# Splitting the first chunk's x right behind attention, and multiplying its rms norm in behind the gate product and h

## The reference

```python
attn = softmax(mask(q @ k.T / 8)); x = attn @ v          # heads 0-3: last 32 keys; 4-7: every 32nd key
rms = sqrt(mean(x * x, -1) + 1e-6)
xn = x / rms * rms_g
g = xn @ w_gate                                          # 512 x 1536
x = (g / (1 + exp(-g)) * (xn @ w_val)) @ w_out           # 1536 x 512
logits = x @ gate + modality_bias[modality_id]           # 8 experts, top 1
out = prob * (relu(x @ w1[e]) @ w2[e])
```

## Time and profile before

| | us |
|---|---|
| median of 3 runs | 973.58 (973.51 to 975.59) |
| the profiled execution | 974.21 |
| its span in the trace | 972.5 |
| TensorE busy | 895.7 |
| DVE, ACT, POOL busy | 434.2, 375.2, 314.7 |

### The profile page before, as it was taken

The page is one execution under the profiler, slowest core; times in us unless marked ns, Lnnn a source line. Parts: engine busy times, 40 slices in busy tenths (PEclk is TensorE's granted clock), DMA queues, the critical chain, the costliest instruction groups (busy, mean ns, idle before and its releaser), DMA issues.

```text
span 972.5 us, 15470 instructions
## 1 busy us (share of the span) xinstructions
PE 895.7 (92%) x5270; PEld 772.6 (79%) x5270; DVE 434.2 (45%) x1120; ACT 375.2 (39%) x952; POOL 314.7 (32%) x375
## 2 busy tenths in 40 slices
PE   6869999999999998999999999992599999999996
PEld 5647888888878886889899989982488888888885
DVE  4644544533454334432533252227374665453651
ACT  4654653544554345521221321122253443333430
POOL 2543575224423442254234222221211222222220
PEclk9999999999999998999999999995699999999999
DMA  9931321321214200211121111112653556242420
GB/s 217 260 98 39 96 50 49 91 70 57 60 33 121 58 23 22 66 33 44 33 76 33 44 65 44 33 34 109 238 209 113 185 205 212 78 161 90 151 98 24
DMA packets 68644, 90.46 MB, mean 93 GB/s; under 512 B 38557, under 2 KB 42653, under 8 KB 68576
## 3 DMA queue, kind: packets, MB, share of 16 engines
q1 hardware_dynamic: 64896, 78.31, 26.5%
q0 software_dynamic: 3680, 11.28, 3.5%
HBM read 80.13 MB, written 10.22 MB: 93 GB/s over the span
## 4 chain that ended last, share of the span: by engine, by line
PE 84%; DVE 6%; ACT 4%; issue 2%; DMA 2%; POOL 1%; SPq 0%; DVEq 0%; POOLq 0%; ACTq 0%
PE ps L718 32%; PE ps L755 13%; PE ps L1272 12%; PE ps L1293 12%; PE ps L670 3%; PE ps L699 3%; PE ps L646 2%; PE ps L1304 2%; PE ps L680 2%; PE ps L775 1%; PE ps L1281 1%; DMA w_raw<-in_moe_w 1%; ACT sm L859 1%; PE ps L766 1%; ACT L865 1%
## 5 line engine op out<-in xcount | busy, mean ns | idle before, releaser
L1001 DVE SCALAR_TENSOR_TENSOR h<-h,ps 128x384 f32<-128x384 f32 x72 | 39.9, 554 | 191.5 <-ACT h L882 191.5
L553 POOL TENSOR_TENSOR sm<-sm,rinv 72x288 f32<-72x288 f32 (+1 forms) x52 | 51.7, 994 | 223.2 <-DVE rinv L964 223.1
L718 PE MATMUL ps<-x_hi,gate_hi 128*128 128x384 f32 x288 | 105.8, 367 | 4.7 <-DVE h L1001 4.7
L718 PE MATMUL ps<-x_hi,val_hi 128*128 128x384 f32 x288 | 102.7, 356 | 0.0
L718 PE MATMUL ps<-x_hi,gate_lo 128*128 128x384 f32 x288 | 98.7, 343 | 0.0
L718 PE MATMUL ps<-x_lo,gate_hi 128*128 128x384 f32 x288 | 98.6, 342 | 0.0
L718 PE MATMUL ps<-x_lo,val_hi 128*128 128x384 f32 x288 | 97.2, 338 | 0.0
L718 PE MATMUL ps<-x_hi,val_lo 128*128 128x384 f32 x288 | 97.1, 337 | 0.0
L581 POOL CAST out_hi<-out_raw 128x512 fp32r<-128x512 f32 x72 | 45.8, 636 | 154.8 <-DMA out_raw<-in_moe_w_out 154.8
L583 POOL TENSOR_TENSOR out_lo<-out_raw,out_hi 128x512 fp32r<-128x512 f32 x72 | 93.6, 1300 | 5.8
L755 PE MATMUL ps<-out_hi,h_hi 128*128 128x512 f32 x216 | 89.7, 415 | 2.4 <-DVE h_lo L1012 2.4
(11 more groups left out here) (196 smaller groups left out, 1908.1 us busy)
## 6 DMA issues: line engine op xcount, KB each, us to landing
w_raw<-in_moe_w SPq DMA_DIRECT2D x64, 512.0 KB, 7.2
out_raw<-in_moe_w_out SPq DMA_DIRECT2D x72, 256.0 KB, 2.6
x_rows<-y_tiles SPq DMA_DIRECT2D x18, 256.0 KB, 2.4
gate_raw<-in_moe_w_gate SPq DMA_DIRECT2D x4, 768.0 KB, 7.0
val_raw<-in_moe_w_val SPq DMA_DIRECT2D x4, 768.0 KB, 7.0
qk<-in_q SPq DMA_DIRECT2D x8, 288.0 KB
qk<-in_k SPq DMA_DIRECT2D x8, 288.0 KB
vstr<-in_v SPq DMA_DIRECT2D x8, 288.0 KB
```

The costliest lines, as they stand in the source:

```text
L553: pool.tensor_tensor(s3, s3, rinv[0:n, i, :].unsqueeze(2).to_broadcast([n, 4, c]), ALU.mult).then_inc(s_no, 1)
L718: mm = pe.matmul(ps[:, bank, 0:CH], w[:, i, kk, cols], x[:, kk, :], start=(kk == 0 and n == 0), stop=(kk == KT - 1 and n == 2))
L1001: dve.scalar_tensor_tensor(out=hf[n % 2][:, :], in0=hf[n % 2][:, :], scalar=1.0, in1=ps[:, 0, 0:CH], op0=ALU.add, op1=ALU.mult).then_inc(s ...
```

## The change

For the first chunk alone, x isn't normalised. Right behind the evacuation of O (ticks 8, 12, 14, 15) ACT casts xT times the gain to x_hi and DVE subtracts to x_lo. The norm goes into a tile of its own (nr_0) and DVE multiplies it in twice per step of chunk 0: on the gate product ahead of tanh (norm_gate), and on h (in form_h). The early stretch has 16 ticks, so the turn of group 13, values 12 and 13 and all behind lie beside products; O of groups 12 to 15 goes to bank 7, the scores of groups 12 to 15 all use banks 5 and 6, and the sum of squares is made at the start of val's product of f = 0, with the norm chain one tick later. The pairs of x are taken in the order 2, 3, 0, 1 everywhere. The gain's load has a semaphore of its own.

```diff
-EARLY = 18
+EARLY = 16
-SS = {0: EARLY - 2, **{c + 1: at(c, 9, 2) for c in range(NC - 1)}}
+SS = {0: at(0, 0, 1), **{c + 1: at(c, 9, 2) for c in range(NC - 1)}}
+X_SPLIT_0 = {2: 8, 3: 12, 0: 14, 1: 15}
+X_SPLIT_AT = by_tick((kk, s) for kk, s in X_SPLIT_0.items())
...
         def score_banks(j):
-            return 0 if SCORE[j] < EARLY and j % 2 else 5
+            return 0 if j < HEAD - 4 and j % 2 else 5
...
             def score(j):
-                elif j >= 2:
-                    pe.wait_ge(s_m, 4 * j - 4)
+                else:
+                    former_user = max((i for i in range(j) if score_banks(i) == bank), default=-1)
+                    if former_user >= 0:
+                        pe.wait_ge(s_m, 4 * former_user + 4)
...
             def product(bank, wh, wl, f, half, done, new=None):
-                for kk in range(half * KT // 2, (half + 1) * KT // 2):
+                for o in range(half * KT // 2, (half + 1) * KT // 2):
+                    kk = ORDER[o]
...
             def gate_product(c, f, half):
                     if c == 0 and f == 0:
-                        pe.wait_ge(s_m, 4 * SCORED[EARLY])
+                        pe.wait_ge(s_m, 4 * (HEAD - 4))
...
+            def x_split_0(kk):
+                if kk == ORDER[0]:
+                    act.wait_ge(s_gain, 16)
+                act.wait_ge(s_oe, last_of_first_chunk(kk) + 1)
+                act.activation(xh[:, kk, :], xT[:, kk, x_cols(0)], ACT.Copy,
+                               scale=rms_gain[:, kk:kk + 1]).then_inc(s_xh, 1)
...
             def tanh(n):
+                if n < FT:
+                    act.wait_ge(s_si, n + 1)
+                    if n:
+                        act.wait_ge(s_gf, n)
+                    act.activation(th_0[:, :], hf[n % 2][:, :], ACT.Tanh, scale=0.5).then_inc(s_th, 1)
+                    return
...
-                if (sub, half) == (1, 0):
+                if (sub, half) == ((2, 0) if (c, f) == (0, 0) else (1, 0)):
                     tanh(FT * c + f)
...
                 for j in EXPS_AT.get(s, []):
                     exps(j)
-                if s == EARLY - 1:
-                    x_split(0)
+                for kk in X_SPLIT_AT.get(s, []):
+                    x_split_0(kk)
...
+            def x_split_0(kk):
+                dve.wait_ge(s_xh, ORDER.index(kk) + 1)
+                dve.scalar_tensor_tensor(out=xl[:, kk, :], in0=xT[:, kk, x_cols(0)], scalar=rms_gain[:, kk:kk + 1],
+                                         in1=xh[:, kk, :].bitcast(f32), op0=ALU.mult,
+                                         op1=ALU.subtract).then_inc(s_xl, 1)
...
+            def norm_gate(n):
+                dve.wait_ge(s_g, n + 1)
+                if n >= 2:
+                    dve.wait_ge(s_hl, n - 1)
+                    dve.wait_ge(s_y, n - 1)
+                dve.tensor_tensor(hf[n % 2][:, :], ps[:, 0, 0:CH], nr_0[:, :], ALU.mult).then_inc(s_si, 1)
+            def form_gate(n):
+                dve.wait_ge(s_th, n + 1)
+                dve.scalar_tensor_tensor(out=hf[n % 2][:, :], in0=th_0[:, :], scalar=1.0, in1=hf[n % 2][:, :],
+                                         op0=ALU.add, op1=ALU.mult).then_inc(s_gf, 1)
...
             def form_h(n):
-                dve.wait_ge(s_si, n + 1)
+                dve.wait_ge(s_gf if n < FT else s_si, n + 1)
...
+                if n < FT:
+                    formed.then_inc(s_hn, 1)
+                    dve.wait_ge(s_hn, n + 1)
+                    formed = dve.tensor_tensor(hf[n % 2][:, :], hf[n % 2][:, :], nr_0[:, :], ALU.mult)
+                formed.then_inc(s_hf, 1)
...
                 if (sub, half) == (1, 0):
-                    scale_gate(FT * c + f)
+                    if c:
+                        scale_gate(FT * c + f)
+                    elif f:
+                        norm_gate(f)
+                if (c, sub, half) == (0, 1, 1):
+                    if f == 0:
+                        normalise_x(0)
+                        norm_gate(0)
+                    else:
+                        form_gate(f)
                 if (sub, half) == (2, 0):
+                    if (c, f) == (0, 0):
+                        form_gate(0)
                     form_h(FT * c + f)
...
                 for val, i in SPLIT_AT.get(s - 1, []):
                     w_lo(val, i, splits)
-                if s == EARLY - 1:
-                    x_split(0)
+                for kk in X_SPLIT_AT.get(s, []):
+                    x_split_0(kk)
```

More of the change, by code:

```diff
@@ L404, in last_batch, with last_of_first_chunk @@
             return (CH * c + CH - 1) // S
+        def last_of_first_chunk(kk):
+            return max(i for i, (hp, g) in enumerate(GROUPS) if hp == kk and (hp >= 2 or g < 2))
         def step_of(s):
@@ L556, in square @@
             def square(c, kk):
[L558 to L561, removed]
+                last = NG * last_batch(c) + LAST[kk] if c else last_of_first_chunk(kk)
+                pool.wait_ge(s_oe, last + 1)
+                if c == 1 and kk == ORDER[0]:
+                    pool.wait_ge(s_n3, 1)
+                elif c and kk == ORDER[0]:
+                    pool.wait_ge(s_xn, KT * (c - 1))
                 x = xT[:, kk, x_cols(c)]
@@ L713, in product @@
                 i, cols = f // QF, slice(f % QF * P, (f % QF + 1) * P)
-                for kk in range(half * KT // 2, (half + 1) * KT // 2):
+                for o in range(half * KT // 2, (half + 1) * KT // 2):
+                    kk = ORDER[o]
                     if new is not None:
-                        pe.wait_ge(s_xl, KT * new + kk + 1)
+                        pe.wait_ge(s_xl, KT * new + o + 1)
                     for n, (w, x) in enumerate(((wh, xh), (wh, xl), (wl, xh))):
                         mm = pe.matmul(ps[:, bank, 0:CH], w[:, i, kk, cols], x[:, kk, :],
-                                       start=(kk == 0 and n == 0), stop=(kk == KT - 1 and n == 2))
+                                       start=(o == 0 and n == 0), stop=(o == KT - 1 and n == 2))
                 if half:
@@ L868, in root @@
                 act.activation(nr[:, :], nr[:, :], ACT.Exp, scale=-0.5).then_inc(s_root, 1)
+            def x_split_0(kk):
[4 more added lines that the diff above has]
+                               scale=rms_gain[:, kk:kk + 1]).then_inc(s_xh, 1)
             def x_split(c):
[L871 to L874, removed]
+                act.wait_ge(s_vp, FT * c)
+                for o, kk in enumerate(ORDER):
+                    act.wait_ge(s_xn, KT * (c - 1) + o + 1)
                     act.activation(xh[:, kk, :], xT[:, kk, x_cols(c)], ACT.Copy).then_inc(s_xh, 1)
             def tanh(n):
+                if n < FT:
[4 more added lines that the diff above has]
+                    return
                 act.wait_ge(s_g, n + 1)
@@ L983, in normalise_x @@
                 dve.wait_ge(s_n2, c + 1)
-                dve.scalar_tensor_tensor(out=nr[:, :], in0=nt[:, :], scalar=1.5, in1=nr[:, :],
+                dve.scalar_tensor_tensor(out=(nr if c else nr_0)[:, :], in0=nt[:, :], scalar=1.5, in1=nr[:, :],
                                          op0=ALU.add, op1=ALU.mult).then_inc(s_n3, 1)
                 dve.wait_ge(s_n3, c + 1)
-                for kk in range(KT):
+                for kk in ORDER if c else ():
                     x = xT[:, kk, x_cols(c)]
@@ L990, in normalise_x @@
                                              in1=nr[:, :], op0=ALU.mult, op1=ALU.mult).then_inc(s_xn, 1)
+            def x_split_0(kk):
[3 more added lines that the diff above has]
+                                         op1=ALU.subtract).then_inc(s_xl, 1)
             def x_split(c):
[L993 to L994 removed]
+                for o, kk in enumerate(ORDER):
+                    dve.wait_ge(s_xh, KT * c + o + 1)
                     dve.tensor_tensor(xl[:, kk, :], xT[:, kk, x_cols(c)], xh[:, kk, :].bitcast(f32),
                                       ALU.subtract).then_inc(s_xl, 1)
+            def norm_gate(n):
[8 more added lines that the diff above has]
+                                         op0=ALU.add, op1=ALU.mult).then_inc(s_gf, 1)
             def scale_gate(n):
@@ L1004, in form_h @@
             def form_h(n):
-                dve.wait_ge(s_si, n + 1)
+                dve.wait_ge(s_gf if n < FT else s_si, n + 1)
                 dve.wait_ge(s_vp, n + 1)
-                dve.scalar_tensor_tensor(out=hf[n % 2][:, :], in0=hf[n % 2][:, :], scalar=0.5, in1=ps[:, 1, 0:CH],
-                                         op0=ALU.mult, op1=ALU.mult).then_inc(s_hf, 1)
+                formed = dve.scalar_tensor_tensor(out=hf[n % 2][:, :], in0=hf[n % 2][:, :], scalar=0.5,
+                                                  in1=ps[:, 1, 0:CH], op0=ALU.mult, op1=ALU.mult)
+                if n < FT:
[3 more added lines that the diff above has]
+                formed.then_inc(s_hf, 1)
             def h_split(n):
```

19 lines of the change are left out of this document (12 added, 7 removed).

## The result

The changed kernel takes 984.75 us (median of 4 runs, 983.39 to 985.68), the kernel before 973.81 in the same comparison: ratio 1.0107, interval 1.0093 to 1.0120. That is +10.9 us where +5.2 was forecast, outside the range.

A forecast was written before the change was run, and what follows sets the result against it. TensorE, busy 92% of a 972.5 us span, was taken as the bound. 2.9 up to f = 1, 2.0 for the clock and 0.3 for chunk 0's rest gave +5.2 us, 978.8 us, range 974.3 to 981.8.

The forecast's parts named there:

- Part 1: Early stretch, ticks 8 to 15: new splits delay DVE's copies at ticks 9 and 13, +2.2 us each, 4.4 in all.
- Part 2: Early stretch two ticks shorter: sum of squares starts at 75.35, where it was 61.88, and no longer waits for POOL.
- Part 3: Norm beside f = 0's products: DVE's chain releases the q/k turn ahead of f = 1 at 87.7 against 84.82, +2.9 us.
- The wait for norm_t: TensorE ahead of values 15: val half 0 covers 2.0 of 3.2 us, 1.2 stay idle.
- Part 4: TensorE clock: f = 1 starts at 1.2 GHz after bursts with gaps; slow products cost +2.0 us.
- The number of slow products: In f = 1: 14 products at the slow clock, 0.15 us more each.
- The upper bound: Clock cost at most 3.4 us, for 23 slow products, as from 72.3 to 80.3 in the kernel before.
- the first rival: Clock rises inside f = 0, near 73.5: +1.8 us in all, 975.4; chance 0.17.
- Part 5: Chunk 0 behind f = 1: two DVE multiplications per step, h 0.6 us later, +0.3 us over eleven steps.
- The early rise of the clock: Clock up inside f = 0: clock term 0, +2.9 becomes +1.5, total 975.4; chance 0.17.
- The absorbed waits: Early waits at ticks 9 and 13 never reach TensorE: 4.4 us back, +0.8, 974.4; chance 0.18, not slower.
- DVE as the bound of chunk 0: Norm on h, two SBUF inputs beside POOL, delays each maximum: +6 over +5.2, 984.5; chance 0.10.

The follow-up runs named there:

- experiment 1: Kernel after with DVE's four early subtractions (x_lo) at the end of the next tick, behind copies and maximum: 978.49 us, ratio 1.0035.
- experiment 7: Kernel after with gate_lo for f = 3 behind the maximum of group 17, not ahead of form_gate of f = 0: 984.40 us, ratio 1.0108.
- experiment 2: Kernel after with 12 and 14 unused products put into TensorE's two waits, ahead of values 15 and the turn before f = 1: 983.15 us, ratio 1.0081.
- experiment 3: Kernel after with chunk 1's four multiplications of x behind the norm on the gate product of f = 10: 982.79 us, ratio 1.0077.
- experiment 4: Kernel after without the norm on chunk 0's gate from f = 1 on, norm on h kept, output different: 977.94 us, ratio 1.0025.
- the four kernels: Kernel after with three, five, four or seven instruction moves on DVE, ACT and TensorE: 974.34, 973.88, 974.84, 973.93 us; ratios 0.9977, 0.9979, 0.9994, 0.9992.
- the kernel of five moves: Kernel after with x_lo, weight splits, chunk 1's multiplications and values 15 later, and the step-end maximum ahead of h_lo: 973.88 us, ratio 0.9979.
- that of three moves: Kernel after with early x_lo a tick later, weight splits two ticks later, chunk 1's multiplications behind f = 10's gate norm: 974.34 us, ratio 0.9977.

## Why the prediction was right in direction and wrong in size

*Part 1, the early waits (+4.4).* Right, in place and size: the copies came at 35.82 and 51.52 (forecast 36 and 51.3), and experiment 1 gives 5.3 us back, 4.8 for the two and the rest for ticks 14 and 15. The second wait is the longer one, since that subtraction took 0.96 us and not 0.6.

*Part 2.* Right. The first product at 66.13 (65.5), the sum of squares at 75.55 (75.4), without POOL.

*Part 3 (+2.9).* Measured 2.6, and DVE was the late one. Inside it one term was wrong: gate_lo was taken at 1.75 us on the path, experiment 7 shows 0.5, since ACT's tanh comes from behind the exponentials and would have been late by itself. That the sum came out so near was in part luck: a path that it didn't have ends only 0.5 us ahead of the one it had. The wait for norm_t was 2.44 and not 1.2, because the clock had risen: val's first product started 0.46 us behind the start of the sum of squares, and val half 0 was through 1.52 us later, at 77.53.

*Part 4, the clock (+2.0).* Mechanism right, 2.8 us measured, 2.7 of it by experiment 2; with experiment 3's execution it would be 1.4, so the size is not a fixed one. The number of slow products, 14, was met: from 87.86 to 93.17. The upper bound counted 23 such products ahead of 80.3 in the kernel before, where its rows have 18, so it should have been 2.7 and not 3.4. The course was another one: I had it low throughout, it rose in f = 0 (the first rival's condition) and fell again behind the waits. That rival's result, a faster f = 1, did not come. The Trainium skill (TensorE: Matmul & The Clock Gate, "HAM oscillation — how this bites in real kernels") describes this: waits between bursts make the clock fall and each new burst pays for it. The rows agree in part: with the waits filled the level stays (experiment 2), but not every wait of 2.4 us or more made it fall (last section).

*Part 5, the rest of chunk 0 (+0.3).* This is the step that failed: 6.1 us, and it is nearly all of the difference between +5.2 and +10.9. I had priced the two multiplications by the slack of one chain, that of h in step 2, and had taken the new order of the gate as free because bank 0 comes free sooner. It was the other way round: the gate's norm costs 4.7 of the 6.1 (experiment 4), and the norm on h 1.5 by itself. The change makes ACT's tanh wait for DVE, and ACT's list carries copies and evacuations that TensorE waits for. Wherever DVE has a long piece of work ahead of norm_gate or form_gate (chunk 1's norm at f = 10, the splits of weights), this now stops three engines. The step that I had looked at, f = 2, has neither.

*The rivals.* The early rise of the clock: its condition came, its time didn't. The absorbed waits: experiment 1 refutes them. DVE as the bound of chunk 0 was priced at 984.5 (its +6 in the place of the +0.3), and 984.75 came out, with a chance of 0.10; that the two agree is luck, since it had nothing for the gate. Its place was half right. The long durations of two-input instructions beside POOL are there (form_gate 523 to 1656 ns over twelve steps, the norm on h 557 to 967), but on the gate's side, and the largest single wait is one of order. The rule of the Trainium skill (SBUF — State Buffer, "Who interferes with whom"), two SBUF inputs of DVE against a reading GpSimd, fits the rows at f = 6: form_gate ends 0.4 us after POOL's cast has. No run takes POOL's work away, so that POOL is the cause is read from the rows and not shown.

What stays open: 0.6 of the 1.5 us that chunk 0 loses with the norm on h alone, how the gate's 4.7 us divide between order and the long instructions beside POOL, and the worth of moving chunk 1's multiplications by itself, which was hidden by the clock.

## What to carry to other kernels

When a value is moved from one engine's chain into another's, list what stands *behind* the new wait on each in-order engine, at every step and not at a typical one: here a multiplication of 0.56 us stood behind 2.2 us of other work on DVE, ACT's tanh waited for it, the copy behind the tanh was late, and TensorE stood for 2.6 us. A producer and consumer pair on two engines belongs a tick apart: moving four subtractions one tick later gave back 5.3 us at the turn ahead of f = 1, where 2.6 had been lost. And work taken off the critical path must be weighed with what it adds: with its order mended the change is level with the kernel before, within about 0.2% (0.9977 to 0.9994; the intervals of two of the four kernels end just under 1, those of the other two take it in). Except for root, the moves were not tried on the kernel before.

## What was not expected of the hardware

A TensorE wait of about 2.5 us can lower the clock for several microseconds, or not. In the kernel after it fell with the wait of 2.44 us that ends at 79.97 and not with the one of 2.61 at 179.94. In experiment 3 it fell with 2.47 at 172.31, in the kernel of five moves with 2.73 at 164.82, in that of three moves it stayed up with 2.69 at 166.01. It can fall with a shorter one too: 1.82 at 172.16 in experiment 7, where 1.80 at 173.34 in the kernel after left it up. The same idle time costs 0 to nearly 3 us more.

The granted clock shows in the totals. In the 24, 23 and 29 runs of the kernel before beside the experiments, those with a mean granted clock of 0.968 or less took 977.8, 978.5 and 977.6 us on average, those with 0.972 or more 972.8, 973.0 and 973.7.
